# The mixer's product over tokens: the last 64 tokens' high and low parts stacked on the partitions, two products in place of three

## The reference

```
h = max(x @ w_in, 0);  u, v = h[..., :512], h[..., 512:]
v_n = (v - mean(v)) / sqrt(var(v) + 1e-6)            # over the 512 channels
v_s = einsum('ts,bsd->btd', w_spatial, v_n) + b_spatial[None, :, None]
out = (u * v_s) @ w_out2
```

## Time and profile before

| | |
|---|---|
| median of 3 runs | 512.09 us (510.92 to 513.74) |
| the profiled execution | 510.92 us |
| its span, first to last instruction | 509.1 us |
| mean granted TensorE clock | 0.990 |
| PE busy | 480.2 us (94%) |
| DVE, ACT, POOL busy | 345.7 (68%), 331.2 (65%), 246.4 (48%) us |

### The profile page before, as it was taken

One profiled execution on the slowest core, in us unless ns is written; L12 is line 12 of the kernel. 1 busy time (PEld: TensorE's weight loads), 2 busy tenths in 40 slices (PEclk: granted clock), 3 DMA queues, 4 the chain that ended last, 5 costly groups with the idle time before them and its releaser, 6 DMA issues.

```text
span 509.1 us, 10189 instructions
## 1 busy us (share of the span) xinstructions
PE 480.2 (94%) x3312; PEld 444.2 (87%) x3312; DVE 345.7 (68%) x823; ACT 331.2 (65%) x879; POOL 246.4 (48%) x246
## 2 busy tenths in 40 slices
PE   2599899689999999999999999999999999999997
PEld 1487687589889999999889999999889999998997
DVE  7777788978777787666577686585577775555140
ACT  4899788947877747766777567676777565434222
POOL 4566464265698554345776455245776341114000
PEclk9999999969999999999999999999999999999999
DMA  6665544744443321543243332532333201200002
GB/s 202 205 181 139 151 120 118 199 106 118 133 108 103 96 72 48 154 130 95 71 118 85 83 95 68 151 107 78 95 96 95 70 14 36 71 1 1 1 0 94
DMA packets 46566, 49.73 MB, mean 98 GB/s; under 512 B 24817, under 2 KB 29073, under 8 KB 46514
## 3 DMA queue, kind: packets, MB, share of 16 engines
q1 hardware_dynamic: 46514, 49.09, 35.8%
HBM read 25.82 MB, written 4.95 MB: 60 GB/s over the span
## 4 chain that ended last, share of the span: by engine, by line
PE 83%; DVE 7%; issue 3%; POOL 2%; DMA 2%; ACT 1%; SPq 1%; DVEq 0%; POOLq 0%
PE mix L1029 45%; PE attn_o L997 9%; PE turned L988 8%; PE score L970 5%; PE score L1029 4%; PE attn_o L1029 4%; PE score L971 4%; DVE u_t L886 2%; DVE prob L849 2%; PE score L977 1%; PE score L978 1%; DMA raw<-in_k 1%; DVE pt_lo L858 1%; DVE act_b L391 1%; ACT prob L707 1%
## 5 line engine op out<-in xcount | busy, mean ns | idle before, releaser
L716 ACT ACTIVATE pt_hi<-turned 128x128 fp32r<-128x128 f32 (+4 forms) x160 | 66.0, 434 | 80.7 <-PE turned L988 80.3
L858 DVE TENSOR_TENSOR pt_lo<-turned,pt_hi 128x128 fp32r<-128x128 f32 (+4 forms) x160 | 74.2, 479 | 48.1 <-ACT pt_hi L716 47.0
L707 ACT ACTIVATE prob<-prob,neg_max 128x128 f32<-128x128 f32 (+4 forms) x160 | 95.2, 600 | 13.3 <-DVE neg_max L849 12.6
L849 DVE CUSTOM_DVE_ANT_0 prob<-score,mask_b 128x128 f32<-128x128 f32 (+4 forms) x159 | 80.6, 534 | 27.3 <-PE score L978 20.8
L988 PE MATMUL turned<-ident,prob 128*128 128x128 f32 (+1 forms) x480 | 64.2, 264 | 14.6 <-DVE pt_lo L858 12.4
L988 PEld LDWEIGHTS turned<-ident,prob 128*128 128x128 f32 (+1 forms) x480 | 51.4, 143 | 28.4 <-issue 22.1
L611 POOL TENSOR_TENSOR q<-raw,raw_hi 64x576 fp32r<-64x576 f32 x31 | 44.7, 1441 | 46.3 <-ACT raw_hi L686 46.3
L427 POOL TENSOR_TENSOR act_b<-u_t,act_b 128x288 fp32r<-128x288 f32 x48 | 38.9, 819 | 50.2 <-ACT act_b L786 44.0
L997 PE MATMUL attn_o<-pt_hi,v_hl 128*128 128x256 f32 (+2 forms) x224 | 62.6, 299 | 0.7 <-DVE pt_lo L858 0.7
L997 PE MATMUL attn_o<-pt_lo,v_hl 128*128 128x256 f32 (+2 forms) x224 | 58.6, 297 | 0.0
L1029 PE MATMUL mix<-ws_hl,act_a 128*128 128x288 f32 (+1 forms) x405 | 57.8, 297 | 0.0
(11 more groups left out here) (147 smaller groups left out, 954.8 us busy)
## 6 DMA issues: line engine op xcount, KB each, us to landing
q<-raw_hi SPq DMA_DIRECT2D x62, 144.0 KB
k<-raw_hi SPq DMA_DIRECT2D x62, 144.0 KB
r_bc<-r_dram SPq DMA_DIRECT2D x32, 144.0 KB, 3.0
out<-work SPq DMA_DIRECT2D x32, 144.0 KB, 2.0
raw<-in_q SPq DMA_DIRECT2D x31, 144.0 KB, 2.7
raw<-in_k SPq DMA_DIRECT2D x31, 144.0 KB, 2.8
v_raw<-in_v SPq DMA_DIRECT2D x32, 128.0 KB, 2.2
u_t<-in_moe_w_in SPq DMA_DIRECT2D x7, 256.0 KB, 3.3
```

The costliest lines, as they stand in the source:

```text
L707: act.activation(prob_view(i), prob_view(i), ACT.Exp, bias=neg_max[p][0:rows[i], i:i + 1], scale=-1.0, accum_out=row_sum[p][0:rows[i], i:i ...
L716: act.activation(pt_view(pt_hi, i), turned_view((g + i) % 2, i), ACT.Copy).then_inc(pt_hi_done, 1)
L849: dve.tensor_tensor_reduce(prob_view(i), score_view(g, i), mask_b[0:rows[i], at:at + width[i]], -SCALE, -LEAST, ALU.add, ALU.min, neg_max[ ...
L858: dve.tensor_tensor(pt_view(pt_lo, i), turned_view((g + i) % 2, i), pt_view(pt_hi, i).bitcast(F32), ALU.subtract).then_inc(pt_lo_done, 1)
```

## The change

The tail's three matmuls become two. The first takes all 128 rows: the activations' high part in rows 0 to 63 and their low part in rows 64 to 127 of plane 0, against the weights' high part in rows 0 to 63 and the same high part again in rows 64 to 127. That is high x high and low x high in one. The second takes 66 rows of plane 1: the activations' high part again with the ones in rows 64 and 65, against the weights' low part with the bias rows. A unit has 14 matmuls.

For this ACT writes the tail's high part a second time in every batch, and the weights' tail once more at the start; the tail's low part goes to partitions 64 to 127 and is written by DVE in all batches, no longer by POOL; one memset per batch on POOL and one in DVE's opening go away. The tail has a semaphore of its own, and the counts of the others' low parts leave it out. `ORDER` is not changed.

```diff
+    TAIL = ("v", NT - 1, 0)
+    LOW = {u: n for n, u in enumerate(u for u in SPLITS if u != TAIL)}
+    NL = len(LOW)
...
-                return v_work(b, n), act_a[0:r, 0, at], act_a[0:r, 1, at]
+                lo = act_a[0:r, 1, at] if n < FULL else act_a[r:2 * r, 0, at]
+                return v_work(b, n), act_a[0:r, 0, at], lo
...
-            eng.tensor_tensor(lo, src, hi.bitcast(F32), ALU.subtract).then_inc(lo_done, 1)
+            eng.tensor_tensor(lo, src, hi.bitcast(F32), ALU.subtract).then_inc(lo_done if unit != TAIL else tail_lo_done, 1)
...
-                sp.dma_start(words(ws_hl[LAST:LAST + 1, 0, tail]), words(wv_hl[0:1, 0, 0:S])).then_inc(b_placed, 16)
-                sp.dma_start(words(ws_hl[LAST + 1:LAST + 2, 0, tail]), words(wv_hl[0:1, 1, 0:S])).then_inc(b_placed, 16)
+                sp.dma_start(words(ws_hl[LAST:LAST + 1, 1, tail]), words(wv_hl[0:1, 0, 0:S])).then_inc(b_placed, 16)
+                sp.dma_start(words(ws_hl[LAST + 1:LAST + 2, 1, tail]), words(wv_hl[0:1, 1, 0:S])).then_inc(b_placed, 16)
...
-                    pool.memset(words(act_a[LAST:LAST + 2, 0, FULL * C:NT * C]), 1.0).then_inc(ones_done, 1)
-                    pool.memset(words(act_a[LAST:LAST + 2, 1, FULL * C:NT * C]), 0.0).then_inc(ones_done, 1)
-                    pool.wait_ge(ones_done, 2 * (b + 1))
+                    pool.memset(words(act_a[LAST:LAST + 2, 1, FULL * C:NT * C]), 1.0).then_inc(ones_done, 1)
+                    pool.wait_ge(ones_done, b + 1)
 
             def split(b, alone, unit):
-                if not alone:
+                if not alone and unit != TAIL:
                     split_lo(pool, b, unit)
...
+                if n == LATE_PIECE + FULL:
+                    act.activation(to[r:2 * r, 0, at:at + length], staged(n), ACT.Copy).then_inc(hi_repeated, 1)
                 act.activation(to[0:r, 0, at:at + length], staged(n), ACT.Copy).then_inc(w_hi_done, 1)
...
                 act.activation(hi, src, ACT.Copy).then_inc(hi_done, 1)
+                if unit == ("v", NT - 1, 0):
+                    act.activation(act_a[0:LAST, 1, FULL * C:NT * C], src, ACT.Copy).then_inc(hi_repeated, 1)
...
-                dve.memset(words(ws_hl[LAST:LAST + 2, 1, FULL * S:NT * S]), 0.0).then_inc(zeroed, 1)
...
             def split(b, alone, unit):
-                if alone:
+                if alone or unit == TAIL:
                     split_lo(dve, b, unit)
...
                 def ready(j):
                     if (m, side) == (0, 0):
-                        pe.wait_ge(lo_done, NS * b + SPLIT[("v", j, 0)] + 1)
+                        pe.wait_ge(*((lo_done, NL * b + LOW[("v", j, 0)] + 1) if j < FULL else (tail_lo_done, b + 1)))
                         if j == NT - 1:
-                            pe.wait_ge(ones_done, 2 * (b + 1))
+                            pe.wait_ge(ones_done, b + 1)
+                            pe.wait_ge(hi_repeated, b + 2)
                             pe.wait_ge(b_placed, 32)
...
-                kr = [P] * FULL + [LAST + 2]
-                return product(mix_tile(b, alone, unit),
-                               [(lambda hl, j=j: act_a[0:kr[j], hl, j * C + m * P:j * C + (m + 1) * P],
-                                 lambda hl, j=j: ws_hl[0:kr[j], hl, j * S + side * HALF:j * S + (side + 1) * HALF])
-                                for j in range(NT)], range(NT), ready)
+                cols_of = slice(FULL * S + side * HALF, FULL * S + (side + 1) * HALF)
+                chans = slice(FULL * C + m * P, FULL * C + (m + 1) * P)
+                o = mix_tile(b, alone, unit)
+                product(o, [(lambda hl, j=j: act_a[:, hl, j * C + m * P:j * C + (m + 1) * P],
+                             lambda hl, j=j: ws_hl[:, hl, j * S + side * HALF:j * S + (side + 1) * HALF])
+                            for j in range(FULL)], range(FULL), ready, False)
+                ready(FULL)
+                pe.matmul(o, act_a[:, 0, chans], ws_hl[:, 0, cols_of], start=False, stop=False)
+                return pe.matmul(o, act_a[0:LAST + 2, 1, chans], ws_hl[0:LAST + 2, 1, cols_of], start=False, stop=True)
```

More of the change, by code:

```diff
@@ L245, in build @@
         lo_done = sem("lo_done")
+        tail_lo_done = sem("tail_lo_done")
         stats_done = sem("stats_done")
@@ L250, in build @@
         ones_done = sem("ones_done")
+        hi_repeated = sem("hi_repeated")
         comb_done = sem("comb_done")
@@ L758, in evict @@
                     if n < NC - 1:
-                        act.wait_ge(lo_done, NS * b + SPLIT[("val", n, 1)] + 1)
+                        act.wait_ge(lo_done, NL * b + LOW[("val", n, 1)] + 1)
                     elif b == 0:
@@ L767, in evict @@
                     if n < NC - 1:
-                        act.wait_ge(lo_done, NS * b + SPLIT[("v", n, 0)] + 1)
+                        act.wait_ge(lo_done, NL * b + LOW[("v", n, 0)] + 1)
                     act.activation(gate(b, unit), mix_tile(b, alone, unit), ACT.Relu).then_inc(clear_act, 1)
@@ L772, in evict @@
                     if n == 0:
-                        act.wait_ge(lo_done, NS * b + SPLIT[("v", NT - 1, 0)] + 1)
+                        act.wait_ge(tail_lo_done, b + 1)
                     if n >= 4:
@@ L881, in tap @@
                         before, m = divmod(NC * b + n - SLOTS, NC)
-                        dve.wait_ge(lo_done, NS * before + SPLIT[("spatial", m, 1)] + 1)
+                        dve.wait_ge(lo_done, NL * before + LOW[("spatial", m, 1)] + 1)
                     dve.tensor_scalar(to, src, w, None, ALU.mult).then_inc(conv_step, 1)
@@ L1002, in pv_first @@
             def pv_first(g):
-                pe.wait_ge(zeroed, 7)
+                pe.wait_ge(zeroed, 6)
                 pe.wait_ge(v_lo_done, g + 1)
@@ L1019, in turn_sums, with product @@
                 pe.transpose(attn_o[0:NT, 0:P], row_inv[g % 2][:, :], ident[:, :]).then_inc(r_turned, 1)
-            def product(o, pairs, part, ready):
+            def product(o, pairs, part, ready, ends=True):
                 for n, (a, b) in enumerate(pairs):
@@ L1029, in product @@
                         ins = pe.matmul(o, a(ha), b(hb), start=(n == 0 and t == 0),
-                                        stop=(n == len(pairs) - 1 and t == 2))
+                                        stop=(ends and n == len(pairs) - 1 and t == 2))
                 return ins
@@ L1071, in ready @@
                     if j in (0, 2):
-                        pe.wait_ge(lo_done, NS * b + SPLIT[("val", kk, j // 2)] + 1)
+                        pe.wait_ge(lo_done, NL * b + LOW[("val", kk, j // 2)] + 1)
                 return product(mix_tile(b, alone, unit),
@@ L1104, in ready @@
                     if m == 0:
-                        pe.wait_ge(lo_done, NS * b + SPLIT[("spatial", kk, side)] + 1)
+                        pe.wait_ge(lo_done, NL * b + LOW[("spatial", kk, side)] + 1)
                 return transposed(b, alone, unit, w2_hl, C, act_b, ready)
```

## The result

| | before | changed |
|---|---|---|
| median of the runs | 512.09 us (510.92 to 513.74, 9 runs) | 509.35 us (507.27 to 510.95, 9 runs) |
| ratio | | 0.994, 95% interval 0.9924 to 0.9956 |
| profiled execution, its span | 510.92, 509.1 us | 509.35, 507.4 us |

A forecast was written before the change was run, and what follows sets the result against it. PE alone was taken to set the time in every spatial unit. 510.92 - 4.24 (32 matmuls) + 0.15 (new wait) = 506.8 us for the profiled execution; by the median 512.09 - 4.1 = 508.0 us, range 505.9 to 510.7 us.

The forecast's parts named there:

- the new wait: First spatial unit, batches 0 to 2: PE waits for DVE's tail low part, 0.05 us each, 0.15 us together.
- 1.5 us for the opening: PE's pause and slow clock before 116 us vary between executions; widens the range by about 1.5 us each side.
- rival A: Tail's low part, slowed beside POOL, stalls PE 0.5 to 1.1 us a batch: 509.4 to 511.2 us; chance 0.12.
- the forecast's own range: Whole kernel, without opening noise or rival A: gain 4.4 to 3.6 us, 507.7 to 508.5 us by the median.
- what bounds, and the price: Spatial units: PE alone sets the time; 32 matmuls less at 0.1325 us, whatever their rows, save 4.24 us.
- nothing for ACT: ACT's second high copy, 0.62 us four times, and repeated weights' copy, 0.67 us, fall in idle time: 0 taken.
- What it pushes on DVE: Taps, first eviction and scores (14, 4) move 0.7 to 0.8 us; PE's third unit is covered by 2.4 us: nothing taken.
- the prediction's own sign: First spatial units: first batch's at the same time as before, later batches' about 1.1, 2.1 and 3.2 us earlier.
- Rival B: DVE becomes what PE waits for, its push paid twice per head, 4.8 to 5.4 us: 513.0 us, slower; chance 0.03.

The follow-up runs named there:

- the side edits alone: Changed kernel with its second tail matmul done twice, so a unit has 15 matmuls as before; 512.77 us, ratio 0.9996 to before.
- the second run: The changed kernel profiled once more, nothing altered; 508.96 us, ratio 0.9922 to the kernel before.
- place 69.3: Changed kernel with VectorE's low part of the last 64 tokens at 69.3, not 69.9, in batches 0 to 2; 508.61, 508.13 and 508.76 us.
- place 70.95: Changed kernel with VectorE's low part of the last 64 tokens at 70.95, not 69.9, in batches 0 to 2; 514.96 us, ratio 1.0041 to before.

## Why the prediction was right or wrong

The measured 509.35 us lies in the range of 505.9 to 510.7 us, and the change is faster, as forecast. The gain on PE came as worked out; up to 0.8 us of it was given back on a path that the prediction had weighed and put at nothing, besides the 0.14 us of the new wait that it had in its sum. The range held because it had 1.5 us for the opening and half of rival A in it: the forecast's own range would have ended at 508.5 us.

**Right: what bounds, and the price.** 32 matmuls were said to be worth 4.24 us; alone they are worth 4.29 (332.15 to 327.86), and 4.25 in the kernels with the corrected place. That the stacked matmul with 128 rows costs no more than one with 66 held: both take 0.14 us in the chain above (187.71 and 187.85 us). A unit of 14 takes 1.58 + 0.14 + 0.14 = 1.86 us.

**Right: the new wait.** "I take 0.05 us for each of three batches": 0.045 us each, 0.14 in all. DVE started the low part at 178.08 in the changed kernel, 0.03 us behind the end of the accumulator read and not beside it, and the tap waited for its end, as the row on L866 had it; this trace agrees with the rule that the prediction cites from the Trainium skill, page "VectorE: DVE Perf Modes", section "Two Vector instructions with no wait between them".

```profile
177.97 0.08 DVE L857 DVE_READ_ACCUMULATOR2_ANT neg_max<- 128x1 f32 x1
178.08 0.69 DVE L433 TENSOR_TENSOR act_a<-work,act_a 64x512 fp32r<-64x512 f32 x1
178.80 1.67 DVE L894 SCALAR_TENSOR_TENSOR u_t<-x_t,taps,u_t 128x576 f32<-128x576 f32 x2
180.39 1.21 DVE L891 TENSOR_SCALAR u_t<-x_t,taps 128x576 f32<-128x576 f32 x1
181.52 0.45 DVE L915 TENSOR_TENSOR u_t<-mix,u_t 128x288 f32<-128x288 f32 x1
```

**Right: nothing for ACT.** From turn (8, 4) to turn (13, 4), where the repeated copy of the weights and the tail's second copy in batch 0 lie, it takes 69.93 us in before, 69.92 in the changed kernel and 69.91 with the side edits alone, by the table (70.51 and 70.50 in the second profiles of before and of the changed kernel). Behind that turn the steady part of the kernel with the low part on GpSimd has no loss with the second copy in place.

**Wrong: the step "What it pushes on DVE".** It had the taps and the first eviction late by 0.7 to 0.8 us, found cover for the third unit, and took nothing. Three things came in its place.

First, the push grew. Against the pace of before (every time 1.63 us later, as turn (13, 4) is) the taps started 0.8 us late. The tap at L883 took 0.52 us before (the earlier trace rows stop short of it) and 1.21 us in the fence above: it now stood beside GpSimd's low part of v, which started at 180.41 us. The first eviction was 1.5 us late, not 0.7 (178.37 us before, 181.52 now).

Second, it was handed on. The sum of a head's two parts (L866 at 185.55 us before, L874 at 187.52 us now) came 0.34 us late against that pace, so GpSimd's division, its q and k parts and two low parts of spatial units were each 0.34 to 0.37 us late, while PE was 0.6 us early at the next turn. GpSimd around 190 us, before and then changed; the last row of each is the pair of low parts:

```profile
189.32 1.41 POOL L613 TENSOR_TENSOR k<-raw,raw_hi 64x576 fp32r<-64x576 f32 x1
190.81 1.57 POOL L427 TENSOR_TENSOR act_b<-u_t,act_b 128x288 fp32r<-128x288 f32 x2
```

```profile
191.29 1.44 POOL L619 TENSOR_TENSOR k<-raw,raw_hi 64x576 fp32r<-64x576 f32 x1
192.81 1.79 POOL L433 TENSOR_TENSOR act_b<-u_t,act_b 128x288 fp32r<-128x288 f32 x2
```

Third, one head later this met DVE's next taps. DVE itself had recovered by then (its turn (14, 4) at 191.27 us moved with PE), but the first two of its three taps now ran beside the later GpSimd pair, where before only the first had, in part. Before, and then changed:

```profile
191.76 0.94 DVE L883 TENSOR_SCALAR u_t<-x_t,taps 128x576 f32<-128x576 f32 x1
192.74 1.67 DVE L886 SCALAR_TENSOR_TENSOR u_t<-x_t,taps,u_t 128x576 f32<-128x576 f32 x2
194.33 0.82 DVE L907 TENSOR_TENSOR u_t<-mix,u_t 128x288 f32<-128x288 f32 x2
```

```profile
192.76 1.17 DVE L891 TENSOR_SCALAR u_t<-x_t,taps 128x576 f32<-128x576 f32 x1
193.97 2.10 DVE L894 SCALAR_TENSOR_TENSOR u_t<-x_t,taps,u_t 128x576 f32<-128x576 f32 x2
195.99 0.81 DVE L915 TENSOR_TENSOR u_t<-mix,u_t 128x288 f32<-128x288 f32 x2
```

From the first tap's start to the eviction it took 194.33 - 191.76 = 2.57 us before and 195.99 - 192.76 = 3.23 us now. The eviction of the fifth unit had been 0.44 us ahead of the seventh unit's first load (194.78 against 195.22); the 0.66 us that the taps lost and the 0.13 us of the sixth unit's missing matmul use that up and leave 0.35 us of idle time, in batch 0 and again in batch 1, or less where the two engines meet a little otherwise (0.17 and 0.17 in the second run). This is PE's wait in the chain at the start:

```profile
196.49 0.83 PEld L1037 LDWEIGHTS mix<-ws_hl,act_a 128*128 128x128 f32 x6 [0.36 <-DVE u_t L915]
```

That the push does it is shown: alone it brings 0.54 us back, and with the low part at place 69.3 or on GpSimd it is gone. That the taps are longer because of GpSimd is read from the traces' coincidences, and was not isolated. The coincidence is a close one: of the 16 taps of the form of L891 in the changed kernel's trace, the six that meet no GpSimd instruction take 0.50 to 0.52 us, and the ten that do take 0.60 to 1.21 us; in before nine take 0.50 to 0.52 us without one, and seven 0.50 to 1.12 us with one. So rival A was right in kind, a part of the gain given back in new waits, but neither in size nor in place: it asked for 0.5 to 1.1 us in each of three batches, and the two profiles have 0.96 and 0.50 us in all; and apart from 0.14 us it came not at the low part but at the seventh unit, two steps behind it.

The wait also shows in the prediction's own sign. Against the first unit it expected the first units of the next batches 1.1, 2.1 and 3.2 us earlier than before; they came 0.6, 1.2 and 2.2 us earlier.

**A reading that was wrong.** Rival A took the 0.91 us of L391 at 123.19 us for the time without a GpSimd instruction. GpSimd was at work there too, and it was GpSimd's pair that was longer, 2.09 us where the same pair takes 1.57 in the fence at 190.81 us:

```profile
122.67 2.09 POOL L427 TENSOR_TENSOR act_b<-u_t,act_b 128x288 fp32r<-128x288 f32 x2
```

**The sum in the profiled executions.** Steady part: 332.15 - 4.25 + 0.14 + 0.8 = 328.84, measured 328.86. The opening: the changed kernel's was 1.63 us later, before's two profiles having caught early ones. So of the 3.29 us only 1.57 are left between the two profiled executions (510.92 and 509.35); 0.09 us lie in neither part. Working back from medians on one chip, an estimate, puts turn (13, 4) at 512.9 - 332.15 - 4.95 = 175.8 us in before and at 508.61 - 327.90 - 5.2 = 175.5 us in the kernel with the low part at place 69.3, where 4.95 and 5.2 us are what their profiled executions have outside these two parts: a shift of the usual opening between the kernels is not seen. The prediction's allowance of 1.5 us for the opening was about right: in the 14 profiles turn (13, 4) lies between 173.8 and 178.2 us.

A small term is in no sum: an execution of before is 1.8 us longer than its span, and one of the changed kernel 2.0 us (2.0 to 2.2 in the other kernels with the side edits). This takes some 0.2 us of the gain; no run shows why.

**Rival B** was given 0.03, rightly for this place in the queue. The run with place 70.95 shows that PE does wait for a late low part: three instructions further back in DVE's queue, and the kernel is slower than before by 0.4%.

**What stays open.** Why turn (8, 4) came at 103.6 to 104.6 us in four profiles and at 105.2 to 107.5 in ten. Between two of them the step comes near 66 us: the same k part on GpSimd takes 1.42 us where it starts early, and 2.23 us where it starts 0.9 us later (GpSimd's q part ahead of it had already started 1.0 us later, at 65.75 against 64.72 us), here first the early and then the late opening:

```profile
66.53 1.42 POOL L619 TENSOR_TENSOR k<-raw,raw_hi 64x576 fp32r<-64x576 f32 x1
```

```profile
67.47 2.23 POOL L621 TENSOR_TENSOR k<-raw,raw_hi 64x576 fp32r<-64x576 f32 x1
```

What decides between them was not found.

## What to carry to other kernels

Where PE's list of waits is empty, a matmul less was worth its distance from start to start, to 1% here, and its row count (66 or 128) did not enter. What is moved to another engine for it should go into that engine's own idle stretch and not beside the first use: 0.6 places earlier in VectorE's queue than the changed kernel has it was free, 1.05 places later cost 5 to 6 us more than the changed kernel. When an engine without gaps is pushed, follow it for a whole period of the schedule, with the second engine that shares its inputs, and compare the slack there with how much earlier PE will be; checking the next consumer alone missed 0.3 to 0.8 us here.

## What the runs showed that was not expected

A push of 0.8 us on VectorE became 1.5 us within three instructions: the tap at L883/L891 took 0.52 us in one position against GpSimd's and 1.21 us in the other. And one kernel's executions differ by up to 6 us (510.0 to 516.0 in 22 runs of before on one chip), while its steady part of 332 us came out the same within 0.02 us in both of its profiles.
